# Two requests and one turn moved at both ends of the routed stage

## The chip, the cores and the metric

One core of one Trainium2 chip. The metric is the device time of one execution in microseconds. A core has five engines with instruction queues of their own: TensorE (PE), VectorE (DVE), ScalarE (ACT), GpSimd (POOL) and SyncE (SP), and 16 DMA engines that all queues share.

## The reference

The input goes through three parts, and only the last is touched here.

1. A linear attention with decay over 2 x 8 heads, 768 steps, head dimension 48. Its output is x, 1536 tokens of 384 values.
2. A dense mixture: 8 experts, each `relu(x @ w1[e]) @ w2[e]` (384 to 1024 to 384), summed with weights from eight rounds of row and column normalisation.
3. A routed mixture: every token goes to the one expert that its cosine scores choose.

```
logits = xn @ en.T / tau
expert_idx = np.argmax(logits, axis=1)
gate_w = probs[np.arange(N), expert_idx]
for e in range(E):
    mask = expert_idx == e
    h = np.maximum(x[mask] @ w1[e], 0.0)
    out[mask] = gate_w[mask, None] * (h @ w2[e])
```

## The kernel before, in words

The program has blocks that follow one another (attention, to_channels, dense_experts, routed_experts). Inside a block the engines run separate streams joined by semaphores; between blocks all engines meet at a barrier.

**End of the dense block (L1062 to L1099, L1198 to L1246).** The last expert's last four tiles of 128 tokens (t = 8 to 11) are finished one after another. For each, PE turns the tile (`turn_tile`) and forms the scores (`score`) and the rank among tokens of the same expert (`rank`). DVE picks the expert (`choose`), computes the gate weight (`weigh`, which ends in the `reciprocal` into column DM of `out` and raises `s_gate`) and the target row in the DRAM table `rows` (`locate`, which writes `pos_i` and raises `s_pos`). For all tiles but the last, POOL then scatters the tile's 128 rows of 388 values to `rows` by an indirect DMA (L785 to L793, over `UNITS[:-1]`). For tile 11 DVE runs `locate` before `weigh`, so the last thing it does in the block is the reciprocal of L1032. The first 128 rows of the first routed slot are put together on PE without DRAM (`first_rows`), so slot 0 needs no load before its products.

**The routed block (L1293 to L1656).** `rows` holds for each expert a region of rows. The work is cut into 19 slots of 128 rows: one for each of the 8 experts, and 11 spare ones that a small table of expert numbers (`slot_table`, DVE) hands out. Each engine's `body(s, q)` runs for s = 0 to 20 (`over_slots`: four written out, a loop of 14, then 18, 19 and 20 written out), q = s mod 2; `there(s)` says whether slot s exists. In slot s:

- SP (`load`, L1393): loads the slot's rows into `m_x`, then w1 of slot s into `raw[1-q][0]`, then w2 of slot s-1 into `raw[q][1]`. SP begins with `sp.wait_ge(s_scat, 16 * TT)`: all twelve scatters have landed. The weights of slots 0 and 1 were loaded in the dense block. The buffers `raw1` (that is `raw[1]`) exist only from the routed block on, in memory that the dense block used.
- PE (`body`, L1640): `hidden(s)`, 18 products x @ w1 in three terms each of a high and a low part (L1612); `turn_x(s+1)`, 3 transposes (L1598); `outward(s-1)`, 24 products h @ w2 (L1636); `turn_hidden(s)`, 8 transposes (L1623). Slot 0 has `hidden(0)`, `turn_hidden(0)`, `turn_x(1)` alone.
- ACT (L1473): the high part of the turned h of slot s-1 (`hidden_hi`, L1471), the high parts of w1 of slot s+1 in four pieces (L1452) with the relus of slot s (L1467) between them, the high part of x (L1463), four pieces of w2 (L1459). In slot 18 the four w2 pieces stand ahead of the second relu.
- DVE (L1541): `finish(s-2)` (y = acc times gate, L1539), `hidden_lo(s-1)` (L1528), then the low parts of w1, x and w2 (L1504, L1519, L1511), each a subtraction from what ACT wrote.
- POOL (L1438): the indirect store of y for slot s-2 (L1434). Ahead of that, POOL's stream in this block begins with the scatter of tile 11 (L1418), and four constants for the slot table (L1421 to L1426).

```
if there(s - 2):
    if there(s - 4):
        sp.wait_ge(s_w1, s - 3)
    load_matrix(sp, w1, KD, e, raw[1 - q][0], s_raw[1 - q][0])
```

PE's `hidden(s)` waits for `s_xlo` (the low part of x, DVE) and `s_w1` (the low part of w1, DVE). `turn_x(s)` waits for the load of `m_x`. `outward(s)` waits for `s_hlo` (both parts of h) and `s_w2`. At the very end POOL waits for the last two stores and the program ends.

Of the kernel before, what the change touches and what calls it, by code (L numbers as in the profile page):

```python
# [614 lines left out]
def dense_experts(nc, w1, w2, x_hi, x_lo, probs, out, raw, hi, lo, s_raw, logits, row_max, ident, ones,  # L615
# [16 lines left out]
    with ExitStack() as ctx:  # L632
# [125 lines left out]
        @block.gpsimd  # L758
        def _(pool):
            def split(e, q):  # L760

                for c, m, a, b in PIECES:
                    pool.wait_ge(s_whi, (e - 1) * NP + c + 1)
                    pool.tensor_tensor(lo[q][m][:, a:b], raw[m][:, a:b], hi[q][m][:, a:b].bitcast(F32),  # L764
                                       ALU.subtract).then_inc(s_wlo, 1)

            pool.memset(out[:, :, 0:DM], 0.0).then_inc(s_zero, 1)
            pool.iota(out[:, :, DM + 1].bitcast(I32), pattern=[[P, TT]], base=0, channel_multiplier=1).then_inc(s_rconst, 1)
            pool.memset(out[:, :, DM + 2:ROW], 0.0).then_inc(s_rconst, 1)
            pool.memset(again[:, :], 1.0).then_inc(s_rconst, 1)  # L770
            pool.wait_ge(s_rconst, 3)
            pool.memset(again[:, 0:GT * E:E], 0.0).then_inc(s_rconst, 1)
            pool.iota(seen[0][:, :], pattern=[[REGION // P, E]], base=0, channel_multiplier=0,
                      allow_small_or_imprecise_dtypes=True).then_inc(s_rconst, 1)
            pool.iota(slot_expert[:, :], pattern=[[1, SLOTS]], base=0, channel_multiplier=0).then_inc(s_rconst, 1)
            pool.iota(slot_row[:, :], pattern=[[REGION, SLOTS]], base=0, channel_multiplier=0).then_inc(s_rconst, 1)
            pool.iota(row_no[:, :], pattern=[[1, P]], base=0, channel_multiplier=0,
                      allow_small_or_imprecise_dtypes=True).then_inc(s_rconst, 1)
            with pool.Fori(0, E // 2 - 1) as i:
                split(i * 2 + 1, 1)  # L780
                split(i * 2 + 2, 0)
            split(E - 1, 1)
            split(E, 0)
            pool.wait_ge(s_fill, 16 * (E + 1))
            for u, (a, b) in enumerate(UNITS[:-1]):  # L785
                pool.wait_ge(s_gate, u + 1)
                pool.wait_ge(s_pos, u + 1)
                if u == 2:
                    pool.wait_ge(s_first, 16)
                for t in range(a, b):  # L790
                    pool.indirect_dma_start(
                        out=rows, out_offset=bass.IndirectOffsetOnAxis(ap=pos_i[:, t:t + 1], axis=0),
                        in_=out[:, t, :], in_offset=None).then_inc(s_scat, 16)  # L793
# [499 lines left out]
def routed_experts(nc, w1, w2, rows, y, ident, ones, filler, slot_expert, slot_row, seen_all, experts_known, s_scat, raw, hi, lo, s_raw,  # L1293
# [10 lines left out]
    with ExitStack() as ctx:  # L1304
# [77 lines left out]
        @block.sync  # L1382
        def _(sp):
            sp.wait_ge(s_scat, 16 * TT)

            def entry(table, s, most):
                at = table[0:1, s:s + 1] if isinstance(s, int) else table[0:1, bass.ds(s, 1)]
                return sp.value_load(at, min_val=0, max_val=most)

            def expert_of(s):  # L1390
                return s if isinstance(s, int) and s < E else entry(slot_expert, s, E - 1)

            def load(s, q):  # L1393

                if there(s):
                    row = s * REGION if isinstance(s, int) and s < E else entry(slot_row, s, E * REGION)
                    one = slice(row, row + P) if isinstance(row, int) else bass.ds(row, P)
                    e = expert_of(s)
                    if there(s - 2):
                        sp.wait_ge(s_meta, s * 2 - 2)  # L1400
                    sp.dma_start(x_in[q][:, :], rows[one, :]).then_inc(s_x[q], 16)  # L1401
                    if there(s - 2):
                        if there(s - 4):
                            sp.wait_ge(s_w1, s - 3)
                        load_matrix(sp, w1, KD, e, raw[1 - q][0], s_raw[1 - q][0])
                if there(s - 1) and there(s - 3):
                    e = expert_of(s - 1)
                    if there(s - 4):
                        sp.wait_ge(s_w2, s - 3)
                    load_matrix(sp, w2, KF, e, raw[q][1], s_raw[q][1])  # L1410
                if isinstance(s, int) and s == 3:
                    sp.wait_ge(experts_known, 2)

            over_slots(sp, load)

        @block.gpsimd
        def _(pool):
            pool.indirect_dma_start(  # L1418
                out=rows, out_offset=bass.IndirectOffsetOnAxis(ap=pos_i[:, TT - 1:TT], axis=0),
                in_=x_tok[:, TT - 1, :], in_offset=None).then_inc(s_scat, 16)  # L1420
            pool.memset(one8[:, :], 1.0).then_inc(s_const, 1)  # L1421
            pool.iota(limit[:, :, :], pattern=[[REGION, E], [P, EXTRA]], base=P, channel_multiplier=0,
                      allow_small_or_imprecise_dtypes=True).then_inc(s_const, 1)
            pool.iota(slot_no[:, :], pattern=[[1, EXTRA]], base=0, channel_multiplier=0,
                      allow_small_or_imprecise_dtypes=True).then_inc(s_const, 1)
            pool.iota(slot_at[:, :], pattern=[[P, EXTRA]], base=P, channel_multiplier=0,  # L1426
                      allow_small_or_imprecise_dtypes=True).then_inc(s_const, 1)
            last_token = pool.to_reg(N - 1)  # L1428

            def put(s, q):  # L1430
                pool.wait_ge(s_tok, s + 1)
                pool.wait_ge(s_yo, s + 1)
                pool.sem_inc(s_go, 1)  # L1433
                pool.indirect_dma_start(  # L1434
                    out=y, out_offset=bass.IndirectOffsetOnAxis(ap=token[q][:, 0:1], axis=0),
                    in_=y_out[q][:, :], in_offset=None, bounds_check=last_token, oob_is_err=False).then_inc(s_put[q], 16)

            def body(s, q):  # L1438
                if there(s - 2):
                    put(s - 2, q)  # L1440

            over_slots(pool, body)
            pool.wait_ge(s_put[0], 16 * ((SLOTS + 1) // 2))
            pool.wait_ge(s_put[1], 16 * (SLOTS // 2))  # L1444

        @block.scalar
        def _(act):
# [25 lines left out]
            def body(s, q):  # L1473
# [17 lines left out]
                if more:  # L1491
                    x_hi(s + 1, 1 - q)
                    if split:
                        w1_hi(s + 1, 1 - q, 3)
                        for c in ON_ACT_HI2:
                            w2_hi(s, q, c)

            over_slots(act, body)

        @block.vector  # L1500
        def _(dve):
# [38 lines left out]

            def body(s, q):  # L1541
                more = there(s + 1)
                if there(s - 2):
                    finish(s - 2, q)
                if there(s - 1):
                    hidden_lo(s - 1, 1 - q, 0)
                    hidden_lo(s - 1, 1 - q, 1)
                split = more and there(s - 1)
                if split:
                    for c in range(NPW - 1):  # L1550
                        w1_lo(s + 1, 1 - q, c)
                if more:
                    x_lo(s + 1, 1 - q)
                if split:
                    w1_lo(s + 1, 1 - q, NPW - 1)
                if there(s) and there(s - 1):
                    for c in ON_ACT_HI2:
                        w2_lo(s, q, c)
# [33 lines left out]
        def _(pe):  # L1592
# [30 lines left out]
                        mm = pe.transpose(hturn[j][:, f * P:(f + 1) * P], h_rows[:, c:c + P], ident[:, :])  # L1623
                    mm.then_inc(s_hturn, 1)

            def outward(s, q):

                if there(s - 2):
                    pe.wait_ge(s_yo, s - 1)
                if there(s - 1):  # L1630
                    pe.wait_ge(s_w2, s)
                for f in range(KF):
                    if f % (KF // 2) == 0:
                        pe.wait_ge(s_hlo, s * 2 + f // (KF // 2) + 1)
                    for x, (a, b) in enumerate(((h_hi, hi), (h_hi, lo), (h_lo, hi))):
                        mm = pe.matmul(acc[q][:, 0:DM], a[q][:, f * P:(f + 1) * P], b[q][1][:, f * DM:(f + 1) * DM],  # L1636
                                       start=(f == 0 and x == 0), stop=(f == KF - 1 and x == 2))
                mm.then_inc(s_acc, 1)

            def body(s, q):  # L1640
                if there(s):
                    hidden(s, q)
                if isinstance(s, int) and s == 0:
                    turn_hidden(s)
                    turn_x(s + 1, 1 - q)
                    pe.wait_ge(s_read, 1)
                    return
                if there(s + 1):
                    turn_x(s + 1, 1 - q)
                if there(s - 1):  # L1650
                    outward(s - 1, 1 - q)
                if there(s):
                    turn_hidden(s)
# [105 lines left out]
```

## Time and profile before

| | us |
|---|---|
| median of 3 runs | 1147.31 |
| lowest, highest | 1147.20, 1147.43 |
| the profiled execution, its own time | 1147.91 |
| its span (first to last instruction) | 1146.2 |
| PE busy in it | 1124.3 (98%) |
| DVE, ACT, POOL busy | 482.1, 438.1, 234.0 |
| DMA moved | 126.07 MB |
| routed block in the span | from 951.4 to the end |

Times in the trace are microseconds from the start of the span; "idle before" is the time in which the engine had nothing running, and the arrow names what ended it. The profiled execution is 0.6 us above the median of the runs and 1.7 us above its own span. PE's ends are modelled: neighbouring products overlap in the record, so a product's pace is read from start to start.

### The profile page before, as it was taken

What the parts mean: (1) busy time and instruction counts of PE and PEld (TensorE: products, weight loads), DVE (VectorE), ACT (ScalarE), POOL (GpSimd) and SP (SyncE); (2) the same over time, 40 slices, a digit from 0 to 9 for tenths busy, and PEclk for the clock granted to TensorE, in tenths of its full rate; (3) what the DMA queues carried; (4) which work ended last, traced back from release to release, by engine and by line L of the source; (5) the groups of instructions that cost most, each with busy time, mean ns of one, the idle gap of its engine ahead of it and who ended that gap; (6) DMA issues with size and microseconds to landing.
All of it is one profiled execution on the core that took longest, in us unless ns stands there. A gap on an engine that the chain in (4) does not pass through costs nothing. (4 is left out here: it accounts for less than half of the span.)

```text
span 1146.2 us, 18279 instructions
## 1 busy us (share of the span) xinstructions
PE 1124.3 (98%) x6881; PEld 1011.5 (88%) x6881; DVE 482.1 (42%) x920; ACT 438.1 (38%) x918; POOL 234.0 (20%) x238
## 2 busy tenths in 40 slices
PE   8999999999999999999999999999999999999997
PEld 6887899999999989999998999999999887999996
DVE  6994552212222221222222122222212465999995
ACT  5776222122122212212221221221123475888884
POOL 5665321022012102201210220121022220111001
PEclk9999999999999999999999999999999999999999
DMA  8420804100500310050031005002000316999991
GB/s 308 150 81 2 284 1 153 42 1 1 194 1 1 141 55 1 1 194 1 1 127 68 1 1 194 1 1 110 2 1 1 138 50 234 372 379 366 358 330 58
DMA packets 61558, 126.07 MB, mean 110 GB/s; under 512 B 3097, under 2 KB 45886, under 8 KB 61488
## 3 DMA queue, kind: packets, MB, share of 16 engines
q1 hardware_dynamic: 59504, 120.30, 29.8%
q0 software_dynamic: 1984, 4.75, 1.1%
q8 instruction: 54, 0.88, 0.3%
q14 instruction: 16, 0.13, 0.0%
HBM read 101.03 MB, written 25.39 MB: 110 GB/s over the span
## 5 line engine op out<-in xcount | busy, mean ns | idle before, releaser
L955 DVE SCALAR_TENSOR_TENSOR h_lo<-hid,h_hi 128x512 fp32r<-128x512 f32 x168 | 116.1, 691 | 497.2 <-ACT h_hi L810 497.2
L810 ACT ACTIVATE h_hi<-hid 128x512 fp32r<-128x512 f32 x168 | 100.5, 598 | 547.4 <-PE hid L1120 547.4
L764 POOL TENSOR_TENSOR w_lo<-raw,w_hi 128x384 fp32r<-128x384 f32 x128 | 129.6, 1013 | 644.7 <-ACT w_hi L802 644.7
L1133 PE MATMUL acc<-w_hi,h_hi 128*128 128x384 f32 x736 | 249.7, 339 | 0.0
L1133 PE MATMUL acc<-w_hi,h_lo 128*128 128x384 f32 x736 | 249.3, 339 | 0.0
L1133 PE MATMUL acc<-w_lo,h_hi 128*128 128x384 f32 x736 | 248.7, 338 | 0.0
L1120 PE MATMUL hid<-x_hi,w_hi 128*128 128x512 f32 x576 | 228.0, 396 | 0.1
L1120 PE MATMUL hid<-x_hi,w_lo 128*128 128x512 f32 x576 | 227.6, 395 | 0.0
L1120 PE MATMUL hid<-x_lo,w_hi 128*128 128x512 f32 x576 | 227.4, 395 | 0.0
L1133 PEld LDWEIGHTS acc<-w_lo,h_hi 128*128 128x128 f32 x736 | 138.2, 188 | 8.5
L1133 PEld LDWEIGHTS acc<-w_hi,h_hi 128*128 128x128 f32 x736 | 138.1, 188 | 7.8
L1133 PEld LDWEIGHTS acc<-w_hi,h_lo 128*128 128x128 f32 x736 | 138.5, 188 | 0.0
L1120 PEld LDWEIGHTS hid<-x_hi,w_lo 128*128 128x128 f32 x576 | 108.5, 188 | 23.9
L1120 PEld LDWEIGHTS hid<-x_hi,w_hi 128*128 128x128 f32 x576 | 108.7, 189 | 18.1 <-issue 0.7
L1120 PEld LDWEIGHTS hid<-x_lo,w_hi 128*128 128x128 f32 x576 | 108.6, 189 | 16.9
L802 ACT ACTIVATE w_hi<-raw 128x384 fp32r<-128x384 f32 x128 | 66.3, 518 | 12.2 <-PE acc L1133 10.7
L1504 DVE TENSOR_TENSOR w_lo<-raw,w_hi 128x768 fp32r<-128x768 f32 x68 | 62.8, 952 | 6.1 <-ACT w_hi L1452 5.1
L1511 DVE TENSOR_TENSOR w_lo<-raw,w_hi 128x768 fp32r<-128x768 f32 x72 | 64.0, 951 | 0.9 <-ACT w_hi L1459 0.9
L985 DVE SCALAR_TENSOR_TENSOR x_tok<-acc,probs,x_tok 128x384 f32<-128x384 f32 x92 | 50.7, 609 | 24.7 <-PE acc L1133 24.7
L1452 ACT ACTIVATE w_hi<-raw 128x768 fp32r<-128x768 f32 x68 | 55.6, 844 | 4.9 <-DMA raw<-in_moe_w 4.9
L1459 ACT ACTIVATE w_hi<-raw 128x768 fp32r<-128x768 f32 x72 | 54.8, 846 | 0.0
L1636 PE MATMUL m_acc<-w_hi,m_hhi 128*128 128x384 f32 x152 | 52.9, 348 | 1.1 <-DVE m_hlo L1528 1.1
(248 smaller groups left out, 1316.5 us busy)
## 6 DMA issues: line engine op xcount, KB each, us to landing
raw<-in_moe_w SPq DMA_DIRECT2D x54, 1536.0 KB, 8.7
rows<-filler SPq DMA_DIRECT2D x8, 2328.0 KB, 16.5
m_x<-rows SPq DMA_DIRECT2D x19, 194.0 KB, 4.7
w_pad<-in_w SPq DMA_DIRECT2D x8, 396.5 KB, 3.5
k_ch<-in_k SPq DMA_DIRECT2D x8, 384.0 KB, 3.5
r_ch<-in_r SPq DMA_DIRECT2D x8, 384.0 KB, 3.6
v_sb<-in_v SPq DMA_DIRECT2D x8, 288.0 KB, 4.9
out_y<-m_y,m_token POOLq DMA_INDIRECT x19, 6.7
```

What stands on the lines that cost most here:

```text
L764: pool.tensor_tensor(lo[q][m][:, a:b], raw[m][:, a:b], hi[q][m][:, a:b].bitcast(F32), ALU.subtract).then_inc(s_wlo, 1)
L802: act.activation(hi[q][m][:, a:b], raw[m][:, a:b], ACT.Copy).then_inc(s_whi, 1)
L810: act.activation(h_hi[st % HB][:, :], hid[st % HB][:, :], ACT.Relu).then_inc(s_hhi, 1)
L955: dve.scalar_tensor_tensor(h_lo[st % HB][:, :], hid[st % HB][:, :], 0.0, h_hi[st % HB][:, :].bitcast(F32), ALU.max, ALU.subtract).then_inc ...
L985: dve.scalar_tensor_tensor(out[:, t, 0:DM], acc[j][:, 0:DM], p, out[:, t, 0:DM], ALU.mult, ALU.add).then_inc(s_out, 1)
L1120: mm = pe.matmul(hid[st % HB][:, :], a[q][0][:, c:c + P], b[:, k, g * GRP:(g + 1) * GRP], start=(k == 0 and x == 0), stop=(k == KD - 1 and ...
L1133: mm = pe.matmul(acc[j][:, 0:DM], a[st % HB][:, j * P:(j + 1) * P], b[q][1][:, f * DM:(f + 1) * DM], start=(f == 0 and x == 0), stop=(f == ...
L1452: act.activation(piece(hi, q, 0, c), piece(raw, 1 - q, 0, c), ACT.Copy).then_inc(s_hi1, 1)
L1459: act.activation(piece(hi, q, 1, c), piece(raw, 1 - q, 1, c), ACT.Copy).then_inc(s_hi2, 1)
L1504: part = dve.tensor_tensor(piece(lo, q, 0, c), piece(raw, 1 - q, 0, c), piece(hi, q, 0, c).bitcast(F32), ALU.subtract)
L1511: part = dve.tensor_tensor(piece(lo, q, 1, c), piece(raw, 1 - q, 1, c), piece(hi, q, 1, c).bitcast(F32), ALU.subtract)
L1636: mm = pe.matmul(acc[q][:, 0:DM], a[q][:, f * P:(f + 1) * P], b[q][1][:, f * DM:(f + 1) * DM], start=(f == 0 and x == 0), stop=(f == KF - ...
```

## The change

Three edits.

1. The load of w1 for slot 2 (into `raw[1][0]`) is taken out of SP's stream and issued by ACT as the first instruction of its stream in the routed block, without a wait.
2. In slot 18, the last, PE no longer runs `outward(17)` whole and then `turn_hidden(18)`. It runs `hidden(18)`, the first half of `outward(17)` (12 products), `turn_hidden(18)`, the second half (12 products). In DVE's body of s = 19 `hidden_lo(18)` comes before `finish(17)` instead of after it.
3. The scatter of tile 11 moves from the head of POOL's stream in the routed block to the tail of POOL's stream in the dense block (`UNITS[:-1]` becomes `UNITS`). It waits there for `s_gate` and `s_pos` to reach 6. SP's wait for all twelve scatters stays.

```diff
-            for u, (a, b) in enumerate(UNITS[:-1]):
+            for u, (a, b) in enumerate(UNITS):
                 pool.wait_ge(s_gate, u + 1)
                 pool.wait_ge(s_pos, u + 1)
...
-                        load_matrix(sp, w1, KD, e, raw[1 - q][0], s_raw[1 - q][0])
+                        if not (isinstance(s, int) and s == 2):
+                            load_matrix(sp, w1, KD, e, raw[1 - q][0], s_raw[1 - q][0])
...
         def _(pool):
-            pool.indirect_dma_start(
-                out=rows, out_offset=bass.IndirectOffsetOnAxis(ap=pos_i[:, TT - 1:TT], axis=0),
-                in_=x_tok[:, TT - 1, :], in_offset=None).then_inc(s_scat, 16)
...
+            load_matrix(act, w1, KD, 2, raw[1][0], s_raw[1][0])
             over_slots(act, body)
...
             def body(s, q):
                 more = there(s + 1)
-                if there(s - 2):
+                last = there(s - 1) and not there(s)
+                if there(s - 2) and not last:
                     finish(s - 2, q)
                 if there(s - 1):
                     hidden_lo(s - 1, 1 - q, 0)
                     hidden_lo(s - 1, 1 - q, 1)
+                if last:
+                    finish(s - 2, q)
...
-            def outward(s, q):
+            def outward(s, q, part=range(KF)):
-                if there(s - 2):
+                if part[0] == 0 and there(s - 2):
                     pe.wait_ge(s_yo, s - 1)
-                if there(s - 1):
+                if part[0] == 0 and there(s - 1):
                     pe.wait_ge(s_w2, s)
-                for f in range(KF):
+                for f in part:
...
-                mm.then_inc(s_acc, 1)
+                if part[-1] == KF - 1:
+                    mm.then_inc(s_acc, 1)
...
                 if there(s):
                     hidden(s, q)
+                if there(s) and not there(s + 1):
+                    outward(s - 1, 1 - q, range(KF // 2))
+                    turn_hidden(s)
+                    outward(s - 1, 1 - q, range(KF // 2, KF))
+                    return
```

## Rows read from the trace of the kernel before

**Rows 1.** The page, busy time by engine: busy us (share), instructions.
```profile
PE 1124.3 (98%) x6881; PEld 1011.5 (88%) x6881; DVE 482.1 (42%) x920; ACT 438.1 (38%) x918; POOL 234.0 (20%) x238
```

**Rows 2.** Chain of waits, start of the routed block: start us, us, what.
```profile
951.41 0.02 POOLq L632
...
952.19 2.74 DMA rows<-x_tok,pos_i
...
955.36 2.63 DMA m_x<-rows
...
958.03 0.55 PE m_turn L1598 x3
...
959.79 5.98 PE m_hid L1612 x18
...
970.34 0.87 PE m_hturn L1623 x8
971.22 4.13 PE m_hid L1612 x18
```

**Rows 3.** Chain of waits, the end of the kernel.
```profile
1129.05 4.20 PE m_acc L1636 x24
1133.25 0.45 PE m_hturn L1623 x4
...
1133.72 0.61 ACT m_hhi L1471
...
1134.35 0.70 DVE m_hlo L1528
...
1140.84 0.02 POOLq L1444
...
1141.05 0.98 POOL out_y L1434
```

**Rows 4.** Timelines of DVE, PE, ACT and SP: start us, us, engine, line [idle before].
```profile
951.01 0.16 DVE L1032 RECIPROCAL x_tok<-esum 128x1 f32<-128x1 f32 x1
```
```profile
956.83 0.66 PE L1623 MATMUL m_hturn<-ident,m_h 128*128 128x128 f32 x4 [0.25 <-ACT m_h L1467]
```
```profile
954.13 0.60 ACT L1467 ACTIVATE m_h<-m_hid 128x512 f32<-128x512 f32 x1 [3.53 <-PE m_hid L1612]
...
964.95 0.85 ACT L1452 ACTIVATE w_hi<-raw 128x768 fp32r<-128x768 f32 x1 [4.87 <-DMA raw<-in_moe_w]
```
```profile
957.98 0.43 SPq L516 DMA_DIRECT2D raw<-in_moe_w  x1
```

**Rows 5.** DMA issues, 951 to 959.3 us: KB each, median us from issue to landing.
```profile
raw<-in_moe_w SPq DMA_DIRECT2D x1, 1536.0 KB, 6.9
m_x<-rows SPq DMA_DIRECT2D x3, 194.0 KB, 2.4
rows<-x_tok,pos_i POOLq DMA_INDIRECT x1, 2.7
```

**Rows 6.** DMA issues, 959.3 to 969 us: m_x asked for behind a matrix.
```profile
m_x<-rows SPq DMA_DIRECT2D x1, 194.0 KB, 5.6
```

**Rows 7.** SP's timeline, and DMA issues from 899.5 to 904.5 us.
```profile
896.56 0.90 SPq L516 DMA_DIRECT2D raw<-in_moe_w  x2
```
```profile
rows<-x_tok,pos_i POOLq DMA_INDIRECT x4, 6.5
```

**Rows 8.** Stretches: length, busy by engine, granted clock, DMA share, GB/s.
```profile
956.93:960.34 3.41, 1.65 (x10) 1.11 (x10) 1.42 (x7) 1.47 (x3) 0.00 (x0) 1.00 0.65 162
960.34:963.75 3.41, 3.41 (x10) 2.65 (x9) 0.67 (x2) 0.00 (x0) 0.00 (x0) 0.51 0.99 391
```

**Rows 9.** Timelines of ACT, DVE and PE in the last slots.
```profile
1130.48 0.58 ACT L1467 ACTIVATE m_h<-m_hid 128x512 f32<-128x512 f32 x1
```
```profile
1128.41 3.56 DVE L1511 TENSOR_TENSOR w_lo<-raw,w_hi 128x768 fp32r<-128x768 f32 x4 [0.93 <-ACT w_hi L1459]
```
```profile
1135.19 0.41 PE L1636 MATMUL m_acc<-w_hi,m_hhi 128*128 128x384 f32 x1 [1.07 <-DVE m_hlo L1528]
```

## The prediction

> **What bounds the kernel now.** I read the page first: PE is busy for 98% of the span [rows 1], so an edit pays only where PE stands still or runs slowly. The chain of waits then says where that is. It follows PE from the end back to 958.0 us through every slot, without a hole between the second slot and the last, so the change can act at two places only: the head of the routed block and its tail.
>
> At the head [rows 2] the chain leaves PE. The barrier is passed at 951.41, POOL's scatter of tile 11 starts at 952.19 and lands 2.74 us later, SP loads the rows of slot 1 (2.63 us from its second request), and at 958.03 PE turns them. PE had been free since 957.49 (956.83 + 0.66) [rows 4]: 0.54 us of waiting for that load. Then 1.21 us (959.79 less 958.03 + 0.55) for ACT's and DVE's two parts of x, and the products of slot 1 start at 959.79. They take 5.98 us where those of slot 2 take 4.13 [rows 2]. The stretches show why [rows 8]: from 956.93 to 960.34 PE was busy for 1.65 of 3.41 us, and in the next 3.41 us the granted clock is 0.51, the lower of its two levels (1.2 GHz instead of 2.4). That costs 1.8 us.
>
> At the tail [rows 3] PE turns h of slot 18 from 1133.25, ACT and DVE split it (0.61 and 0.70), and PE's last products start at 1135.19 after 1.07 us without work [rows 9]. After them come y, the store and the program's end, which the change doesn't touch.
>
> **Edit 2, the tail: -1.0 us.** 24 products take 4.20 us, so half of outward(17) takes 2.10. It starts at 1129.05, ends at 1131.15, and the 8 turns (0.87, [rows 2]) run to 1132.0. The second four turns need ACT's second relu of slot 18, over at 1131.06 (1130.48 + 0.58) [rows 9]: just in time, since they begin at about 1131.6. The second half runs to 1134.1. ACT makes the first high part from 1131.6 to 1132.2, the second some 0.5 later; DVE is busy with w2 until 1131.97 [rows 9], then makes the low parts from 1132.2 to 1133.6 (two of 0.70). Both are there before 1134.1, so the hole of 1.07 is covered; the cover that is left is 0.5 us. One more switch between turns and products costs something below 0.1 (the first product after turns takes 0.41 us in [rows 9]; its start-to-start pace is what counts, and that row doesn't give it; I bound it by 0 and 0.1). finish(17) now waits behind hidden_lo(18) and behind the end of outward(17): y of slot 17 is made 0.9 us later, and its store too. The last store is asked for 5 us after it, so POOL is free again, and nobody else waits. Net -1.0, bounds -1.07 and -0.9.
>
> **Edit 1, w1 of slot 2.** SP loses one request of 0.43 us [rows 4] at 957.98, when nothing behind it is due; 0. ACT gains it at about 951.5, where it stands idle for 3.53 us until its relu at 954.13 [rows 4]; 0. The load moves 6.4 us forward, from 957.98 to 951.55, and ACT's wait of 4.87 us at 964.95 [rows 4] goes. But PE doesn't profit: the products of slot 2 start at 971.22, right behind the turns that end there [rows 2]. What is late next in that stretch is PE itself. The loads behind it on SP's queue come earlier, and PE waits for none of them. So the edit is worth 0 by itself, and what it can do is harm: 1536 KB that take 6.9 us to land alone [rows 5] now travel from 951.55 to about 958.5, beside the scatter and the two row loads of slots 0 and 1, the second of which is on PE's path.
>
> **Edit 3, the scatter.** DVE's last reciprocal ends at 951.17 [rows 4]. POOL's scatter can start then. How soon is not shown for a scatter whose own wait ends last. At the end of the kernel POOL's sequencer was already at the line behind the store (1140.84) before the store itself began (1141.05) [rows 3]: it runs ahead of its engine. So the wait may stand in the engine's queue, with the preparation done: start at 951.35, 0.84 earlier than 952.19. Or the preparation comes after the wait, as between 951.41 and 952.19: start at 951.17 + 0.76 = 951.93, 0.26 earlier, and POOL reaches the barrier some 0.5 us late, which all engines pay. I take the first, nearest to the row of the sequencer. The constants for the slot table stand behind the scatter on POOL in both kernels, and SP needs that table long after; 0.
>
> **The head, both together.** Scatter: 2.7 us to landing with nothing beside it [rows 5], 6.5 behind two matrices in flight [rows 7]. Here the matrix is asked for 0.2 us after the scatter starts, so I take 3.2, near the lower end: 951.35 + 3.2 = 954.55. SP's second request goes out 0.4 later, at 954.95. Alone it lands in 2.6 (957.6); 1.9 us behind a matrix on the same queue a row load took 5.6 [rows 6], which would be 960.6. I take the time at which w1 is through, about 958.7 (958.45, and 0.2 for the scatter's share): 3.7 us. PE turns the rows of slot 1 at 958.7 instead of 958.03: +0.7. The stretch of low clock covers the start of the products of slot 1; if it lies where it did, a delay that pushes work past 960.34 costs half, since the work that leaves the slow stretch runs at the full clock afterwards. So +0.6.
>
> The Trainium skill (DMA: Bandwidth & Descriptors, Queues, rings and completion order) says that each DMA engine takes turns between the queues of SP, ACT and POOL, packet by packet. By that alone the row loads would get half of the traffic, some 2 us of data instead of 1 (0.39 MB at half of about 400 GB/s), and land about 1 us late: near what I take. The 6.5 us of [rows 7], POOL's scatters beside SP's loads, speak against so even a share, and rival C below rests on that row.
>
> **Sum.** Head +0.6, tail -1.0, net -0.4. The profiled execution took 1147.91, 0.6 above the median of the runs, so 1147.5 for a like execution and **1146.9** for the median. About 0.2%, 2.3 us, is what a measurement of this kernel can tell from no change.
>
> **Rivals.**
>
> A is the forecast (own range 1146.0 to 1147.9). Chance 0.50.
>
> B, no harm done: w1 travels beside the small transfers without delaying them. The rows of slot 1 land at 957.1 to 957.4, and PE turns them at 957.49: -0.54. With the tail -1.5: 1145.8, chance 0.18. In that case PE idles less in the stretch ahead of 960.34, and the clock may stay at its upper level; then another 1.8 goes (5.98 against 4.13): -3.3, 1144.0. For it: the stretch before the low clock had PE busy for 1.65 of 3.41 us [rows 8], and 0.54 more would stand in it. Against: the 1.21 us of idling stay. Chance 0.12.
>
> C, slower: the matrix comes first. If ACT's packets are in the DMA engines before the scatter's, the scatter takes 6.5 us instead of 3.2 [rows 7] and lands at 957.9; SP then asks at 958.3 for the rows of slot 1, which land at 960.9 to 961.5, and PE turns them 2.9 to 3.5 us late. With -1.0 at the tail that is +1.9 to +2.5, less if part falls into the slow stretch, and 1.7 more if a second slow stretch follows the longer idling. I price it at +2.5: 1149.8. It decides against the change from a landing of the scatter above about 4.3 us. For it: four scatters in [rows 7]. Against: the two matrices there were asked for from 896.56 on, 3 us and more before the first of them, and here the two requests fall together. Chance 0.15.
>
> D, the tail doesn't do what it says: the second relu of slot 18 comes later and holds the turns, or the parts of h are late. The relu has about 0.5 us to spare. Then the head's +0.6 stands alone: 1147.9. Chance 0.05.
>
> **Chances.** Faster by over 0.2%: B with the upper clock and a little of its neighbourhood, 0.13. Slower: two thirds of C, 0.10. Within: 0.77. The range reaches from B with the full clock to most of C: 1143.9 to 1149.5.
>
> **What would show it.** Tail: no hole before the last products, `hidden_lo(18)` ahead of y of slot 17, last products 1.0 earlier relative to `hidden(18)`. Head: POOL's scatter at 951.35 and PE's first instruction of the block at 951.57 as before (if 0.5 later, the preparation is paid at the barrier); the landing of the scatter at 3.2 rather than 2.7 or 6.5; the rows of slot 1 landing at about 958.7; ACT's first high part of w1 right behind the parts of h, at about 961; the products of slot 2 directly behind the turns. I am wrong if the scatter lands in more than 5 us (C), if PE turns the rows without waiting (B), or if the granted clock in the products of slot 1 stays full.

## The result, and the profile after

The changed kernel takes 1150.91 us in the median of 8 runs against 1147.62 us for the kernel before beside it. The ratio of the two is 1.0024, with a 95% interval of 1.0015 to 1.0033: slower by 2.8 us, clear of noise, just above the 2.3 us that the prediction took as the bound. (The two medians by themselves differ by 3.3 us; what is compared below is the ratio.) The profiled execution took 1149.22 us (span 1147.3) against 1147.91 (1146.2) before, which is less of a loss than the medians show, for a reason outside the change that is given below. A few executions took 47 to 50 us longer, with the clock low for 116 us early in the attention where a trace shows one: the ratios leave them out, the medians do not, and of the traces of e9 and e10, which come from two of them, only the routed block is read.

The chain of waits of the changed kernel at the head of the routed block (start us, us, what):

```profile
949.98 0.02 POOLq L632
...
950.02 7.03 DMA rows<-x_tok,pos_i
...
957.06 0.35 SPq L1401
...
957.47 2.53 DMA m_x<-rows
...
960.05 0.90 PE m_turn L1600 x3
960.95 1.22 issue
962.17 6.04 PE m_hid L1614 x18
...
973.60 4.13 PE m_hid L1614 x18
```

Set beside [rows 2]: POOL's scatter starts 0.04 us after the barrier, where it used to start 0.78 after it (952.19 less 951.41). But it takes 7.03 us to land instead of 2.74. The rows of slot 1 then land as quickly as before (2.53), only too late: PE turns them 10.07 us after the barrier, and before it was 6.62. The timeline of PE shows the wait as PE's own:

```profile
960.05 0.90 PE L1600 MATMUL m_turn<-ident,m_x 128*128 128x128 f32 x3 [3.98 <-DMA m_x<-rows]
```

The DMA issues of the changed kernel from 949 to 962 us (KB each, median us from issue to landing) set beside [rows 5]:

```profile
raw<-in_moe_w ACTq DMA_DIRECT2D x1, 1536.0 KB, 7.3
m_x<-rows SPq DMA_DIRECT2D x3, 194.0 KB, 2.5
rows<-x_tok,pos_i POOLq DMA_INDIRECT x1, 7.0
```

ACT asked for the matrix at 950.10, so it landed at 957.4. The scatter landed at 957.05. The small transfer of 0.2 MB finished with the large one that was asked for 0.1 us after it.

The packets in the trace, queue by queue, show where the time went. The matrix's first packet moved at 951.18, the scatter's first at 955.06, 5.04 us after its start; in the kernel before it came 1.53 us after the start (953.72). Until 955.06 the DMA engines had moved 1.15 of the matrix's 1.57 MB and nothing of the scatter. From then on both moved side by side: from 955 to 956 us the scatter's packets took 43% of the engines' time and the matrix's 59%.

The clock, as busy time by stretch (length, busy by engine, granted clock, DMA share, GB/s), set beside [rows 8]:

```profile
949.98:958.87 8.89, 5.68 (x28) 4.44 (x28) 2.12 (x11) 1.20 (x2) 1.65 (x5) 1.00 0.65 220
958.87:962.28 3.41, 1.01 (x4) 0.64 (x4) 0.99 (x6) 1.29 (x3) 0.00 (x0) 0.50 0.37 121
962.28:965.70 3.42, 3.42 (x8) 2.70 (x9) 1.96 (x3) 0.90 (x2) 0.00 (x0) 0.50 0.74 195
```

The granted clock is at half (1.2 GHz) for 6.83 us instead of 3.41, but its first half falls where PE is mostly idle (busy for 1.01 of 3.41 us). The products of slot 1 take 6.04 us instead of 5.98, and the turns 0.90 instead of 0.55: the longer low stretch costs 0.4 us beyond what the kernel before already paid.

At the tail (chain of waits, set beside [rows 3]) the change does what it says:

```profile
1131.44 2.10 PE m_acc L1638 x12
1133.54 0.87 PE m_hturn L1625 x8
1134.41 4.57 PE m_acc L1638 x26
1138.98 3.05 issue
1142.03 0.02 POOLq L1442
...
1142.24 0.98 POOL out_y L1432
```

From the first product of slot 17's outward part to the last store it is 10.80 us (1142.24 less 1131.44) against 12.00 (1141.05 less 1129.05). The hole of 1.07 us is gone; the "issue" of 3.05 holds no waiting of PE: its last products run to 1140.24, and DVE makes y from 1140.81 to 1141.43.

The span, piece by piece, from these two chains:

| piece | before | after | difference |
|---|---|---|---|
| start to the barrier | 951.41 | 949.98 | -1.43 |
| barrier to the first product of slot 2 (the head) | 19.81 | 23.62 | +3.81 |
| from there to slot 17's outward part | 157.83 | 157.84 | 0.0 |
| the tail, to the last store | 12.00 | 10.80 | -1.20 |
| last store to the end | 5.15 | 5.06 | -0.1 |
| span | 1146.2 | 1147.3 | +1.1 |

The first line has nothing to do with the change: set side by side, the two traces part by 1.55 us between 110 and 130 us, in the attention, where the two programs are the same, and keep that distance, but for 0.1 us, to the barrier. The clock there:

```profile
110.00:130.00 20.00, 17.38 (x84) 12.77 (x82) 10.13 (x26) 9.29 (x21) 11.99 (x17) 0.91 0.59 205
```
```profile
110.00:130.00 20.00, 17.38 (x91) 13.03 (x90) 11.24 (x29) 9.23 (x21) 12.38 (x17) 1.00 0.59 206
```

The first is before (granted clock 0.91), the second after (1.00). The low stretch there (3.41 us at half in the trace before) comes and goes: the traces of the changed kernel, e2 and e7 have none, those of e3, e4 and e6 have one. So one trace against one trace hides 1.4 us. Head and tail alone make +2.6, close to the 2.8 of all runs.

### The profile page after: what moved, and what is told of

It reads as the page before. It is cut to its first block and busy times, and to the rows that moved or that the text cites. A ratio compares the mean times of both kernels' runs of the same rounds, so it can differ in the third digit from the quotient of the medians.

```text
span 1147.3 us, 18280 instructions
## 1 busy us (share of the span) xinstructions
PE 1122.2 (98%) x6881; PEld 1010.2 (88%) x6881; DVE 483.4 (42%) x920; ACT 438.6 (38%) x918; POOL 234.0 (20%) x238
## 3 DMA queue, kind: packets, MB, share of 16 engines
q10 hardware_dynamic: 400, 1.57, 0.4%
## 5 line engine op out<-in xcount | busy, mean ns | idle before, releaser
L1120 PEld LDWEIGHTS hid<-x_hi,w_hi 128*128 128x128 f32 x576 | 108.3, 188 | 18.1 <-issue 0.8
L1432 POOL DMA_INDIRECT out_y<-m_y,m_token x19 | 18.7, 986 | 172.8 <-DVE m_y L1538 162.0
```

The lines of the kernel that those rows point to most:

```text
L1120: mm = pe.matmul(hid[st % HB][:, :], a[q][0][:, c:c + P], b[:, k, g * GRP:(g + 1) * GRP], start=(k == 0 and x == 0), stop=(k == KD - 1 and ...
```

## The experiments

Two theories were set against the scatter's 7 us. T: the matrix that ACT asks for at the barrier holds it back in the DMA engines. P: its new place, with its wait standing in POOL's queue, makes it slow. K was that the clock, not the wait, makes the loss; the chain above speaks against it, since 3.45 of the head's 3.81 us are the later turn and 0.4 are the clock's. Kernels e1 to e4 ran on one chip, with 30 runs of the kernel before (median 1148.05); e5 to e8 on one (25 runs, 1148.21); e9 to e12 on one (32 runs, 1148.15). Ratios compare with the kernel before.

**e1: without ACT's request.**

```diff
-            load_matrix(act, w1, KD, 2, raw[1][0], s_raw[1][0])
...
-                        if not (isinstance(s, int) and s == 2):
-                            load_matrix(sp, w1, KD, e, raw[1 - q][0], s_raw[1 - q][0])
+                        load_matrix(sp, w1, KD, e, raw[1 - q][0], s_raw[1 - q][0])
```

> The changed kernel with w1 of slot 2 asked for by SP again, at its old place; the early scatter and the turned tail stay. Theory T (the matrix that ACT asks for holds back the scatter in the DMA engines): the scatter lands 2.7 us after its start instead of 7.0, PE turns the rows of slot 1 about 6.1 us after the barrier (before: 6.6, changed: 10.1), and the median is 1.2 (tail) and 0.5 (head) below that of before, about 1145.9. Rival P (the scatter is slow because of its new place at the end of the dense block, its wait standing in POOL's queue): the landing stays at 7.0 and the median near 1150.9. Rival K (the low clock, not the wait, makes the loss): the wait goes but a low stretch of 6.8 us stays, 1147 to 1148.

Measured: 1145.83, ratio 0.9980 [0.9971, 0.9988]. T holds and P falls. Its chain, from slot 0 on:

```profile
953.43 4.22 PE m_hid L1612 x18
...
958.33 0.66 PE m_hturn L1623 x4
958.98 0.33 PE m_turn L1598 x3
959.31 1.22 issue
960.53 4.44 PE m_hid L1612 x18
...
970.37 0.38 issue
970.75 4.33 PE m_hid L1612 x18
```

PE turns the rows of slot 1 (958.98) with no wait for them, 6.1 us after the barrier (POOL's scatter starts at 952.95 here). The products of slot 1 run at the full clock: 4.44. Now w1 of slot 2 is late: PE stands for 0.38 us until DVE's last low part of it, over at 970.64. So the early scatter and the turned tail are worth 2.3 us together, and ACT's request turns that into a loss of 2.8: it costs about 5 us. The two heads differ by 5.78 us (23.62 and 17.84). Of this 4.0 are the earlier turn, 2.2 the full clock in turns and products, and the wait for w1 takes 0.4 back. So the clock does not make the loss against the kernel before, but it has a good third of what e1 gains on the changed one.

**e2: without the early scatter.** The scatter stands at the head of POOL's stream in the routed block again.

```diff
-            for u, (a, b) in enumerate(UNITS):
+            for u, (a, b) in enumerate(UNITS[:-1]):
```

> The changed kernel with the scatter of tile 11 back at the head of POOL's stream in the routed block; ACT's request for w1 and the turned tail stay. Theory T: the scatter starts 0.8 us later than in the changed kernel, behind the same matrix, and lands when that is nearly through, 6 to 7 us after its start: median 1151 to 1152. Rival P: the landing is back at 2.7 us, PE turns the rows of slot 1 at 6.6 us after the barrier, median 1146.4. Rival K: low clock of 6.8 us with either landing.

Measured: 1151.69, ratio 1.0035 [1.0021, 1.0048]. The chain shows the old place with the new delay:

```profile
951.44 6.51 DMA rows<-x_tok,pos_i
...
958.37 2.49 DMA m_x<-rows
...
963.02 7.10 PE m_hid L1617 x18
```

P falls a second time, T holds. Here the low stretch is 10.2 us long (958.65 to 968.89) and covers the first 5.9 us of the products of slot 1, which take 7.10.

**e3: the tail alone.** Edits 1 and 3 undone.

> The kernel before with the turned tail alone (half of the products of slot 17, the turns of slot 18, the other half; hidden_lo of slot 18 ahead of finish of slot 17). The changed kernel's trace gives 10.80 us from the first product of slot 17's outward part to the last store, against 12.00 before: all theories expect -1.2, a median of 1146.4, with the head as before. If the tail's gain were given back behind the store (the closing drain of POOL), the median would be 1147.6.

Measured: 1146.73, ratio 0.9986 [0.9977, 0.9994], which is -1.6 by the ratio (-0.7 to -2.6) and -1.3 in the medians. The head is 19.68 us (19.81 before), the tail 10.80. The tail's gain is not given back.

**e4: the matrix behind the rows of slot 1, on SP.**

```diff
                     sp.dma_start(x_in[q][:, :], rows[one, :]).then_inc(s_x[q], 16)
+                    if isinstance(s, int) and s == 1:
+                        load_matrix(sp, w1, KD, 2, raw[1][0], s_raw[1][0])
```

> Early scatter and turned tail, and w1 of slot 2 asked for by SP directly behind the rows of slot 1, ahead of the rows of slot 2 (ACT asks for nothing). Theory T: scatter 2.7 us, rows of slot 1 within 2.6 us as before, since they are ahead of the matrix on their queue; PE turns them without waiting, 6.1 us after the barrier. Median 1145.9, or about 1144 if the clock then stays up in the products of slot 1 (5.98 us before, 4.13 at full clock). Against kernel e1 it differs only if w1 of slot 2 is late there: then it is faster than e1 by that wait. Rival P: 1150.9, since the scatter stands where the change put it.

Measured: 1146.75, ratio 0.9984 [0.9975, 0.9993]; about 1 us short of what was expected. The chain goes through a load that had never mattered:

```profile
956.48 7.62 DMA m_x<-rows
964.10 0.04 issue
964.14 0.55 PE m_turn L1601 x3
```

These are the rows of slot 2, asked for at 956.48, behind the matrix (954.73). PE waits 0.96 us for them; the products of slot 1 ran at the full clock (18 in 4.4 us). Moving the matrix moved the queueing to the next small load.

**e5: ACT asks when the scatters have landed.** One added line, `act.wait_ge(s_scat, 16 * TT)`, ahead of ACT's request.

> The changed kernel with one more wait: ACT asks for w1 of slot 2 only when all scatters have landed, at the moment at which SP asks for the rows of slots 0 and 1. Theory T with a depth (what is asked for later, on whatever queue, waits behind what the DMA engines have already taken in): the scatter is back at 2.7 us; the rows of slot 0 go out with the matrix and land in about 3, those of slot 1, asked for 0.4 us later, in 3 to 7. PE turns the rows of slot 1 up to 4 us late: median 1146 to 1149. If the engines shared evenly between queues, the rows would land about 1 us late and the median be 1146.5. Rival K (low clock): no prediction for the landings.

Measured: 1152.24, ratio 1.0030 [1.0017, 1.0043], as bad as the change and worse than the range given; the even share (1146.5) is out too. The chain:

```profile
954.12 2.73 DMA rows<-x_tok,pos_i
...
956.86 0.35 SPq L1401
...
957.27 7.17 DMA m_x<-rows
...
964.49 0.90 PE m_turn L1601 x3
```

The scatter is back at 2.73, and now the rows of slot 1 take 7.17. Landing times of that line, for the requests at 956.9 and 957.3 us (min/median/max):

```profile
DMA to landing us min/median/max: 2.6/4.9/7.2
```

The rows of slot 0, asked for by SP at the same moment as the matrix by ACT (956.86 and 956.87), land in 2.6; those of slot 1, 0.4 us later, in 7.2. So the delay needs neither POOL nor an indirect DMA nor a write. What counts is the order of the requests, by tenths of a microsecond; which moment of a request counts is taken up below.

**e6: the same early request by SP, ahead of its wait.**

> The changed kernel with the same early request made by SP, ahead of its wait for the scatters, instead of by ACT. Theory T: the queue doesn't matter, the scatter lands 6.5 to 7 us after its start and the median is 1150 to 1152, as in the changed kernel. Rival Q (it is ACT's queue that takes precedence over POOL's): the scatter lands in about 2.7 to 3.5 us, median 1146 to 1147.

Measured: 1151.24, ratio 1.0031 [1.0019, 1.0043]; the scatter lands in 6.86 us. Rival Q falls: the queue that asks makes no difference. The Trainium skill says so too (DMA: Bandwidth & Descriptors, Issuing engines are not separate DMA queues): another issuing engine saves only issue time, and the transfers interleave on the same engines. The two traces (7.03 and 6.86 us) agree.

**e7: a third of the matrix.** ACT asks early for the first third (`raw[1][0][:, 0:F]`, on a semaphore of its own), SP for the rest at the old place.

> The changed kernel with ACT asking early for one third of w1 of slot 2 only (512 KB, one 4096-byte row per partition); SP asks for the other two thirds at the old place. Theory T with a depth: the scatter waits for the packets in front of it, so it is held back by a third of the matrix's time, 3.84 us / 3 = 1.3: landing 3.9 to 4.4 us, PE turns the rows of slot 1 0.5 to 1 us later than before relative to the barrier, median 1146.5 to 1147.5. Rival F (any matrix in flight costs a fixed delay of 4.3 us): landing 7.0, median near 1151. Even shares: landing 3.3 or less.

Measured: 1148.62, ratio 1.0002 [0.9992, 1.0012]. The issues from 948 to 962 us:

```profile
raw<-in_moe_w ACTq DMA_DIRECT2D x1, 512.0 KB, 4.0
rows<-x_tok,pos_i POOLq DMA_INDIRECT x1, 4.6
```

The scatter takes 4.6 us: 1.9 above the 2.7 alone, where the whole matrix adds 4.3. Rival F, a fixed delay, falls, and so does the even share (3.3 or less). The delay grows with the bytes asked for at the same time, though not in proportion, and its size was off (1.2 to 1.7 expected) and the median is above the range given (1146.5 to 1147.5): the low stretch is 6.8 us long here too, and the products of slot 1 take 6.64.

**e8: ACT asks when the rows of slot 0 have landed** (`act.wait_ge(s_x[0], 16)`).

> The changed kernel with ACT's request for w1 of slot 2 held until the rows of slot 0 have landed (ACT waits on that load's semaphore). Then scatter and both row loads are through or nearly so, and w1 comes about 0.5 us earlier than in e1, ahead of the rows of slot 3 only. Theory T: scatter 2.7, rows of slot 1 2.5 to 3, rows of slot 2 (SP, at the same time) up to 6 us, still due later than that; the 0.38 us that PE waited for w1 of slot 2 in e1 go. Median 1145.5, the fastest of the set, against 1145.83 for e1. If the rows of slot 2 fall behind the matrix as in e4 (7.6 us), PE waits for them and the median is 1146.7.

Measured: 1147.10, ratio 0.9990 [0.9981, 0.9999]; a miss by 1.6 us. The transfers are as T says (scatter 2.76, rows of slot 0 2.38), but the chain shows ACT's request standing in front of ACT's relu:

```profile
956.48 0.43 ACTq L516
...
956.96 0.61 ACT m_h L1465
...
957.61 1.15 PE m_hturn L1626 x8
```

PE waits for that relu and the low stretch returns (products of slot 1 5.73). The head is 20.21 us, no shorter than before; what is left of the gain is the tail's.

**e9: ACT asks behind its second relu of slot 0.**

```diff
                 if there(s):
                     relu(s, 1)
+                if isinstance(s, int) and s == 0:
+                    load_matrix(act, w1, KD, 2, raw[1][0], s_raw[1][0])
```

> The changed kernel with ACT's request for w1 of slot 2 placed behind its second relu of slot 0, some 5.3 us after the barrier, when the scatter has landed and the rows of slot 1 are nearly there, and when it holds no relu up (in e8 it held one up by 0.43 us). Theory T: scatter 2.7, rows of slot 1 2.4 to 2.8, PE turns them 6.1 us after the barrier and doesn't wait for w1 of slot 2 (0.38 us in e1). Median level with e1 or 0.4 below it; 1.2 to 2.2 below the kernel before.

Measured: 1145.09, ratio 0.9976 [0.9968, 0.9985], the lowest median of all, 0.24% below the kernel before and, by the two ratios, 0.5% below the changed one. By the ratio that is 2.8 us below the kernel before, where 2.2 was the most that was expected. Its chain:

```profile
1005.02 0.66 PE m_hturn L1626 x4
1005.68 0.33 PE m_turn L1601 x3
1006.01 1.22 issue
1007.23 4.43 PE m_hid L1615 x18
...
1016.32 0.87 PE m_hturn L1626 x8
1017.19 4.13 PE m_hid L1615 x18
```

No wait for the rows of slot 1, none for w1 of slot 2, and only the 1.22 us that were never touched. ACT's request went out at 1004.38, 4.8 us after the barrier. The next small load now stands behind it: the rows of slot 2, asked for at 1005.05, take 6.4 us and land at 1011.5, just as PE comes to turn them (1011.65 in the chain). There is nothing to spare.

**e10: e9 with the idle time of PE filled**, and **e11: the kernel before with it**.

```diff
                     turn_x(s + 1, 1 - q)
+                    for _ in range(2):
+                        pe.matmul(acc[0][:, 0:256], ident[:, :], filler[:, 0:256], start=True, stop=True, skip_group_check=True)
                     pe.wait_ge(s_read, 1)
```

> e9 with two products of the unit matrix and zeros (128x256 each) on PE behind the turns of slot 1, in the 1.22 us in which PE waits for the two parts of x; they write a bank that is overwritten later and lengthen nothing. Theory K2 (the low clock in the products of slot 1 comes from PE's idling ahead of them, and is a term of its own beside the wait): no stretch of low clock in the routed block's head, products of slot 1 in 4.2 to 4.4 us, median up to 1.7 below e9 where e9 has the stretch, equal where it has not. If idling is not what lowers the clock: equal to e9, with the stretch as often.

> The kernel before with the same two products alone. K2: the stretch of 3.41 us at half clock in the products of slot 1 (5.98 us) goes, they take 4.2 to 4.4, median 1.5 to 1.8 below the kernel before. Otherwise within 0.3 of it. This also sizes the clock's share in the loss of the changed kernel, whose low stretch is 6.8 us.

Measured: e10 1145.52, ratio 0.9978 [0.9968, 0.9988], level with e9. That decides little, since e9's trace has no low stretch in the head that filling could remove; in e10's trace PE waits 0.26 us for the rows of slot 2. e11 1147.63, ratio 0.9997 [0.9988, 1.0006]: no difference that can be told, against 1.5 to 1.8 expected. In e11's trace the low stretch is indeed gone and the products of slot 1 take 4.44 (the two added products are the four records of L1647), but:

```profile
958.43 0.86 PE m_acc L1647 x4
959.30 0.35 issue
959.65 4.44 PE m_hid L1612 x18
...
969.49 0.56 issue
970.05 4.37 PE m_hid L1612 x18
```

PE then waits 0.56 us for w1 of slot 2, which SP still asks for late. That leaves -1.06 at the head (18.75 against 19.81) in this trace. The runs give -0.5 in the medians and -0.3 by the ratio, with an interval from -1.4 to +0.7, so that 1.06 is not excluded. That filling the idle time takes the low stretch away rests on this one trace of e11 (the one trace of before and that of e3 have it). How often the low stretch falls on the products of slot 1 without a profile was not measured.

**e12: the kernel of e1 again.**

> The kernel of e1 again (early scatter and turned tail, w1 of slot 2 asked for by SP at its old place), on the same chip as e9 to e11, to compare with them: again 1.5 to 2.3 below the kernel before, scatter 2.7 us, PE waits 0.3 to 0.5 us for w1 of slot 2 where the products of slot 1 run at the full clock, and not at all where they don't.

Measured: 1146.35, ratio 0.9983 [0.9974, 0.9992], with a wait of 0.63 us for w1 of slot 2. e9 beside it is 1.3 lower in the median, though the two intervals overlap, so that e9 beats e1 is likely and not settled.

The head in all traces, in us, from the barrier to the first product of slot 2; the scatter and the rows from request to landing:

| kernel | scatter | rows of slot 1 | products of slot 1 | head |
|---|---|---|---|---|
| before | 2.74 | 2.63 | 5.98 | 19.81 |
| changed | 7.03 | 2.53 | 6.04 | 23.62 |
| e2 | 6.51 | 2.49 | 7.10 | 24.92 |
| e6 | 6.86 | 2.58 | 6.03 | 23.46 |
| e5 | 2.73 | 7.17 | 6.07 | 24.0 |
| e7 | 4.62 | 2.55 | 6.64 | 21.77 |
| e8 | 2.76 | 2.5 | 5.73 | 20.21 |
| e3 | 2.73 | 2.53 | 5.96 | 19.68 |
| e11 | 2.68 | 2.66 | 4.44 | 18.75 |
| e4 | 2.71 | 2.6 | 4.4 | 18.69 |
| e12 | 2.7 | 2.6 | 4.43 | 18.1 |
| e10 | 2.76 | 2.5 | 4.4 | 18.0 |
| e1 | 2.7 | 2.5 | 4.44 | 17.8 |
| e9 | 2.7 | 2.6 | 4.43 | 17.6 |

## Why the prediction was wrong

The forecast was 1146.9 us with a range to 1149.5; the median is 1150.91. It failed at one step, the head, and there at one term. Against the prediction's own sum the scatter landed 3.8 us later after its start (7.03 for 3.2), started 0.1 later, and the rows took 1.2 less (2.53 for 3.7); so PE's turn came 3.45 us late and not 0.7.

- **The scatter's landing, the step that failed.** The prediction took 3.2 us, near the lone 2.7, because the matrix was asked for after the scatter had started and not before it. Measured: 7.03, at the far end of the bounds (6.5 from [rows 7]). What it missed: POOL works on the scatter's instruction for about a microsecond (0.96), ACT on its request for 0.43. Both start at the barrier, the matrix's packets move first, and the small transfer stands behind 1.15 of its 1.57 MB. That the matrix does it, on whatever queue, and the more the larger it is, is shown by e1, e6 and e7, and by e5 for another small transfer. That POOL's 0.96 us lose the race is read from the order in which the issuing instructions end, in the traces where the whole matrix and a small transfer are asked for on different queues within 0.7 us of each other (all in us):

| small transfer | starts after the matrix's request starts | ends after it ends | lands in |
|---|---|---|---|
| e5, rows of slot 0 | -0.01 | -0.09 | 2.6 |
| e8, rows of slot 2 | 0.25 | 0.14 | 5.3 |
| e5, rows of slot 1 | 0.40 | 0.38 | 7.2 |
| changed, scatter | -0.08 | 0.44 | 7.0 |
| e6, scatter | -0.09 | 0.49 | 6.9 |
| e9, rows of slot 2 | 0.67 | 0.57 | 6.4 |
| e10, rows of slot 2 | 0.67 | 0.57 | 6.8 |

By the starts the scatters of the changed kernel and of e6 come first, and are late all the same; by the ends every row fits. No run changes this order alone, so it stays a reading of seven rows.

- **The rows of slot 1.** The prediction put 3.7 us on them, since it thought they would travel beside the matrix. They took 2.53: the scatter had used up the matrix's whole time, and nothing was left for the rows to wait behind. Where the scatter is kept clear and the matrix is asked for with the rows of slot 0 (e5), they take 7.17. In each of these traces only one small transfer of the chain pays, and it pays all of it.
- **Rival C, at 0.15, is what happened.** It gave +2.5 us in all, by a landing of 6.5 and a turn 2.9 to 3.5 late; measured are 7.03, 3.45 and a ratio that makes +2.8. Mechanism, place and price were right, the chance was not. Its point of decision (a landing above 4.3 us) was far exceeded. The remark that spoke against it, that the requests of [rows 7] had come 3 us and more after their matrices, was no argument: e5 has 0.4 us and the full delay. e7 stands near the point of decision from the other side: a landing of 4.62 and a ratio of 1.0002.
- **The even share.** The prediction put beside its estimate the Trainium skill (DMA: Bandwidth & Descriptors, Queues, rings and completion order), by which each DMA engine takes turns between queues packet by packet. By that alone the late transfer would land about 1 us late. It landed 4.3 to 4.7 late, on POOL's queue and on SP's. The packets show both halves of it. For 3.9 us (951.18 to 955.06) only the matrix moves, so the traces do not agree with an even share for a newcomer, and the measurement decides; once the scatter's packets move, the two queues have 43% and 59% of the engines' time, which is near the turn-taking that this section of the Trainium skill states.
- **Edit 3's start was right.** POOL's scatter starts 0.04 us after the barrier, the preparation done, and the barrier is not late. The prediction had it 0.06 us ahead of the barrier (951.35 against 951.41) and 0.18 after the reciprocal's end; measured is 0.28 (949.74 to 950.02).
- **The tail was right**: -1.0 predicted, -1.20 in the trace, -1.3 by e3.
- **Edit 1 is worth nothing by itself: right by the trace of the kernel before, and wrong once the head is shorter.** Where the products of slot 1 run at the full clock and SP asks at the old place, PE does wait for w1 of slot 2: 0.38 us in e1, 0.63 in e12, 0.56 in e11. The edit's aim is real; its moment was wrong. Edit 1 alone was not run.
- **The clock.** A second low stretch came as C had it, but cost 0.4 us and not 1.7, because it fell on idle time. Rival B's full clock did appear where the wait went (e1, e4, e9, e12: 4.4 us for the products of slot 1), so its description is of those kernels, not of the change.

What holds the newcomer's first packet back inside the DMA engines is not shown by these runs; only the order and the amount are.

## What to carry to other kernels

A large load that is moved to an idle moment is not free when a small transfer on the critical path is asked for within the same microsecond: here 1.5 MB that land in 7 us delayed it by 4.3 to 4.7 us, whichever queue asked. Ask for it when the last small transfer of the chain has gone, and then look at the next small load behind it (e4) and at what stands behind the request on its engine (e8). When a trace has one contended example and one lone one, and the change makes the contended case possible, price it by the contended row.

## What the runs showed of the hardware that was not expected

- 0.4 us of order decide over 4.6 us of landing: in e5 the load asked for at 956.86, with the matrix at 956.87, lands in 2.6 us, and the same-sized one at 957.27 in 7.17.
- A third of the matrix delays the scatter by 1.9 us, the whole by 4.3. The scatter's first packet moves 1.53 us after POOL's start alone, 3.06 beside the third (954.54 less 951.48) and 5.04 beside the whole.
- A wait attached to the last indirect DMA of a block costs POOL neither the barrier nor the preparation: POOL's sequencer passes the barrier (949.98) before the scatter starts (950.02), and this is 0.28 us after DVE's reciprocal ended (949.58 + 0.16), where the kernel before needed 0.78 from the barrier to the scatter.
